# Score matmuls of a gated linear attention on 64x32 tiles of TensorE, keys in two parts, without the masked key part of the highest level

## What is computed

```python
def _attn_ref(q, k, v, alpha):
    for t in range(S):
        state = alpha[:, :, t, :, None] * state + np.einsum('bhd,bhe->bhde', k[:, :, t], v[:, :, t])
        y[:, :, t] = np.einsum('bhd,bhde->bhe', q[:, :, t], state)

def _moe_ref(x, domain_probs, w1, w2):      # 4 experts, 384 -> 1024 -> 384
    p = domain_probs / (domain_probs.sum(-1, keepdims=True) + 1e-09)
    for e in range(E):
        out += p[:, e:e + 1] * (np.maximum(x @ w1[e], 0.0) @ w2[e])

def _moe2_ref(x, w_in, w_out):              # 384 -> 2048 -> 384
    h = x @ w_in
    return (h * np.clip(h + 3.0, 0.0, 6.0) / 6.0) @ w_out
```

## Time and profile before

| what | value |
|---|---|
| time, three runs | 1381.57 us median (1380.89 to 1384.29) |
| the profiled execution's own time | 1382.56 us |
| its span in the profile | 1380.6 us |
| TensorE busy | 1356.1 us (98%), 13596 matmuls and as many weight loads |
| VectorE, ScalarE, GpSimd busy | 699.7, 534.8, 790.9 us (51%, 39%, 57%) |
| mean granted TensorE clock | 0.989 |
| DMA | 150.33 MB, mean 109 GB/s |

### The profile page before, as it was taken

The page is one execution under the profiler, slowest core; times in us unless marked ns, Lnnn a source line. Parts: engine busy times, 40 slices in busy tenths (PEclk is TensorE's granted clock), DMA queues, the critical chain, the costliest instruction groups (busy, mean ns, idle before and its releaser), DMA issues.

```text
span 1380.6 us, 34120 instructions
## 1 busy us (share of the span) xinstructions
PE 1356.1 (98%) x13596; PEld 1105.3 (80%) x13596; DVE 699.7 (51%) x1401; ACT 534.8 (39%) x992; POOL 790.9 (57%) x863
## 2 busy tenths in 40 slices
PE   6799999999999999999999999999999999999998
PEld 5578888888888888888888888888888888888887
DVE  8877665444454554454544544454445443333333
ACT  2233334333354333354433344533335433335543
POOL 7877665656565656565656565656564444444442
PEclk7899999999999999999999999999999999999999
DMA  4243343343334433433443334343322343333331
GB/s 146 73 144 119 115 117 117 104 125 95 110 96 126 126 118 103 119 95 114 130 126 104 109 96 126 104 124 112 114 85 85 99 128 106 104 99 92 99 118 35
DMA packets 70667, 150.33 MB, mean 109 GB/s; under 512 B 9584, under 2 KB 22128, under 8 KB 70512
## 3 DMA queue, kind: packets, MB, share of 16 engines
q1 hardware_dynamic: 70512, 148.16, 35.8%
HBM read 143.36 MB, written 4.77 MB: 107 GB/s over the span
## 4 chain that ended last, share of the span: by engine, by line
PE 95%; issue 0%; DVE 0%; ACT 0%; DVEq 0%
PE psum L517 43%; PE psum L501 42%; PE psum L417 5%; PE psum L458 1%; PE psum L438 1%; PE psum L428 1%; PE psum L473 1%; PE psum L481 1%; DVE result L664 0%; DVE psum L644 0%; DVE x_lo L660 0%; ACT gate L779 0%; ACT x_hi L799 0%; DVEq L148 0%; ACT w_hi L792 0%
## 5 line engine op out<-in xcount | busy, mean ns | idle before, releaser
L892 POOL TENSOR_TENSOR w_lo<-w_raw,w_hi 128x768 fp32r<-128x768 f32 (+1 forms) x291 | 531.7, 1828 | 537.2 <-ACT w_hi L792 537.2
L786 ACT ACTIVATE h_hi<-psum 128x512 fp32r<-128x512 f32 x288 | 172.6, 599 | 628.1 <-DVE psum L638 553.3
L517 PE MATMUL psum<-h_hi,w_hi 128*128 128x512 f32 x864 | 344.8, 399 | 0.2 <-DVE x_lo L660 0.2
L517 PE MATMUL psum<-h_hi,w_lo 128*128 128x512 f32 x864 | 337.3, 390 | 0.0
L501 PE MATMUL psum<-x_hi,w_hi 128*128 128x512 f32 x864 | 336.5, 389 | 0.3 <-issue 0.3
L517 PE MATMUL psum<-h_lo,w_hi 128*128 128x512 f32 x864 | 336.7, 390 | 0.0
L501 PE MATMUL psum<-x_lo,w_hi 128*128 128x512 f32 x864 | 336.1, 389 | 0.0
L501 PE MATMUL psum<-x_hi,w_lo 128*128 128x512 f32 x864 | 336.1, 389 | 0.0
L638 DVE SCALAR_TENSOR_TENSOR psum<-psum,probs 128x512 f32<-128x512 f32 x192 | 134.2, 699 | 349.4 <-PE psum L501 349.3
L792 ACT ACTIVATE w_hi<-w_raw 128x768 fp32r<-128x768 f32 x288 | 241.4, 838 | 0.0
L650 DVE TENSOR_TENSOR h_lo<-psum,h_hi 128x512 fp32r<-128x512 f32 x288 | 197.3, 685 | 46.5 <-ACT h_hi L786 46.5
(11 more groups left out here) (52 smaller groups left out, 717.4 us busy)
## 6 DMA issues: line engine op xcount, KB each, us to landing
w_raw<-w SPq DMA_DIRECT2D x288, 384.0 KB, 3.1
alpha_q<-qa SPq DMA_DIRECT2D x48, 256.0 KB, 3.8
k_raw<-kk SPq DMA_DIRECT2D x48, 128.0 KB, 3.7
probs<-prob_scratch SPq DMA_DIRECT2D x24, 256.0 KB, 3.6
v_diag<-v SPq DMA_DIRECT2D x96, 48.0 KB, 2.5
out<-result SPq DMA_DIRECT2D x18, 256.0 KB, 4.0
level_sb<-level SPq DMA_DIRECT2D x1, 80.0 KB, 3.2
ident_sb<-ident SPq DMA_DIRECT2D x1, 64.0 KB, 2.9
```

The costliest lines, as they stand in the source:

```text
L517: mm = pe.matmul(out_bank[k], a, x[:, g % DEEP, :], start=first and i == 0, stop=last and i == 2)
L786: act.activation(h_hi[:, g % DEEP, :], h_bank[g % 2][:, :], ACT.Copy).then_inc(hh_made, 1)
L892: op = pool.tensor_tensor(w_lo[:, g % RING, cols], w_raw[:, g % RAW, cols], w_hi[:, g % RING, cols].bitcast(F32), ALU.subtract)
```

## The change

In `score`, each matmul whose stationary operand was 64 keys becomes two, of 32 keys each, on the output quarters `quarter(jj, 0)` and `quarter(jj, 1)`: 64 rows by 32 columns of the array instead of 64 by 64, with the same moving operand. At level 5 the second part (keys 32 to 63, which the mask leaves out) is not made, from chunk 2 on; for chunks 0 and 1, the first to write the two pairs of banks, it is. A chunk has 88 score matmuls instead of 48 (96 in chunks 0 and 1). What `keep` reads is unchanged. Nothing else is edited.

```diff
                 for l in range(LEVELS):
                     at, width = ((0, CH // 2), (CH // 2, CH))[l] if l < 2 else (CH // 2 * (l + 1), CH // 2)
+                    parts = 2 if l < LEVELS - 1 or n < 2 else 1
                     for jp in range(2):
                         for i in range(2):
                             for jj in range(2):
...
                                 lo = 512 * i + SLAB * jp + at
-                                mm = pe.matmul(j_out[own(jj), lo:lo + width], k_level(n, l)[own(i), j, :], moving,
-                                               start=True, stop=True)
+                                for half in range(parts):
+                                    mm = pe.matmul(j_out[quarter(jj, half), lo:lo + width],
+                                                   k_level(n, l)[own(i), j, 32 * half:32 * half + 32], moving,
+                                                   start=True, stop=True)
                 mm.then_inc(p_made, 1)
```

## The result

The changed kernel takes **1455.7 us** (median of four runs, 1451.48 to 1460.06) against 1382.05 us in as many runs of the kernel before: a ratio of 1.053 (95% interval 1.051 to 1.055). It is slower, by 73.6 us. The profiled execution has a span of 1457.7 us, 77.1 more than before. The four runs fall in two pairs (1451.5 and 1451.9, 1459.6 and 1460.1 us), and the profiled one is of the upper pair, so sums from its trace come out some 4 us above the median.

The account below looks back on a forecast made before the run. The prediction took TensorE, busy 98% of the span, to bound the kernel. Against the profiled 1382.56 us it summed -8 + 39 + 20 + 6 = +57 to 1439.6, so 1438 us for the median, range 1400 to 1475.

Parts of the forecast that it names:

- pace of 40 bursts: Main loop score bursts: 176 records at 6.5 to 6.7 ns save 0.2 us per chunk, 40 chunks, -8 us.
- stops for code, main loop: Main loop: TensorE waits for code when two block borders lie in one score burst, +39 us (ends 27 and 51).
- half clock, main loop: Main loop: after each of 12 stops of 2 us or more, 3.4 us at half rate, +20 us (ends 0 and 41).
- prologue: Prologue: rounds grow from some 366 to 526 instructions; 1 us for each of six rounds, +6 us (ends 0 and 14).
- One block ahead and no more: TensorE's code fetch: the next 256-instruction block's packet starts only once the block before it is entered.
- the ramp: Main loop chunks 9, 13, 16, 28, 29, 41, 42: first border at position 101 to 131, partial stops of 0.8 to 2.3 us.
- code is fetched in time: Rival: no waits for code, only the pace is left, 1381.6 - 8 = 1373.6 us; chance 0.08.
- X: Time from entering a code block to using the next: taken as 4.2 us in the main loop, ends 3.5 and 5.0.
- VectorE and GpSimd and the filler matmuls hide much of it: Prologue: other work covers most of 8.4 us of code fetching a round, leaving 1 us for each of six rounds.
- 6.5 ns: Time per record read from L458's 32 records of 64x32 tiles in the main loop, applied to the new score bursts.
- the tile's columns set the pace: Score bursts: 64x32 tiles start records faster (6.5 ns) than 64x64 tiles (14.6 ns); moving columns do not matter.
- The tiles don't overlap in this order: Rival: four matmuls in a row on the same 64 rows, 13.3 ns a record, 2.3 us a burst, 1460 us; chance 0.08.

Follow-up runs that it names:

- e2: Changed kernel with 52 tiny matmuls on zeros (208 instructions) between prologue and main loop, moving only the code-block borders: 1425.2 us (one run).
- e3: Changed kernel with 20 tiny matmuls on zeros (80 instructions) between prologue and main loop, moving only the code-block borders: 1477.0 us (one run).
- e4: Changed kernel with 64x32 tiles only from chunk 8 on, the prologue's eight chunks as before the change: 1405.4 us (one run).
- e8: Changed kernel with the masked key part of the highest level computed as well, 192 records a burst: 1495.1 us (one run).
- e6: Changed kernel with the score burst cut in two around 18 large matmuls from chunk 16 on, earlier chunks on 64x64 tiles: 1400.2 us, ratio 1.0125.
- e5: Changed kernel with 64x32 tiles in the prologue's eight chunks alone, main loop on 64x64 tiles as before: 1401.6 us (one run).
- e7: Kernel before, with only the highest level on 64x32 tiles and its masked key part left out, from chunk 2 on: 1383.42 us, ratio 1.0006.
- e1: Changed kernel with the order inside a level turned so consecutive score matmuls alternate between the two row halves: 1461.66 us (one run).

## Why the prediction was right, and which terms were not

The direction and the cause held: 1438 us was said (the sum gives 1438.6) with 1400 to 1475, and 1455.7 came. The slowdown was put at 57 us and is 74. The two large terms, both of the main loop, were right; the other two missed by 14 and 15 us, both to the same side. Term by term, as the sum had them:

| term | said | measured | from |
|---|---|---|---|
| pace of 40 bursts | -8 | +6 | 1.68 us instead of 1.53, x 40 |
| stops for code, main loop | +39 | +36 | 16 gaps |
| half clock, main loop | +20 | +19 | 37.5 us at half rate |
| prologue | +6 | +21 | 94.5 instead of 73.7 us |

The measured ones add to 82, for 77 of the span; part of the low clock falls into stops, where it costs nothing. The same sum, with each run's own numbers, gives the main loop's extra time in the others (us over the 1301.9 of before):

| kernel | stops, over 1 us | stops, us | low clock, us | stops + half of it + burst | measured |
|---|---|---|---|---|---|
| changed | 13 | 35.8 | 37.5 | 60 | 56 |
| e2, moved by 208 | 4 | 10.3 | 10.2 | 21 | 20 |
| e3, moved by 80 | 20 | 50.4 | 41.0 | 77 | 73 |
| e4, main loop only | 4 | 9.3 | 13.7 | 22 | 22 |
| e8, masked part kept | 20 | 55.8 | 68.3 | 101 | 94 |

**Code: right.** One block ahead and no more, a stop when two borders lie in one burst, and the chunks by counting: 11, 15, 25 to 27 and 37 to 40 all have theirs, and of the seven on the ramp 13, 16, 28, 29, 41 and 42 do, the later ones in the turn or the large matmuls behind the burst. Chunk 9 has none and 14 has one of 0.9 us that was not named. The border is 256 instructions and not the work: e2, e3 and e4 moved the stops by count, and e6 removed them. One block ahead shows at all 16 stops: no further packet had started when TensorE went on, and the next one started 1.2 to 4.2 us later. By the rule set beside the rival "code is fetched in time" no burst of 352 would wait; in the main loop eight were cut. X, the time from entering a block to the use of the next, was near the middle: a full stop took 2.0 to 3.6 us where 3.2 was said. Its packet time of 1.65 us came from one packet; at these stops it was 0.9 to 1.4.

**Clock: right in sum.** Some stops over 2 us were followed by 3.4 us at 1.2 GHz, some by 6.8, and some, above all those near 2 us, by none. The term was half the stretch of one row of the prologue, and that it met is partly luck; e3 shows the spread.

**Prologue: the step that failed most.** It said that "VectorE and GpSimd and the filler matmuls hide much of it", 1 us a round. The stops fell in the scores, once a round, 2.1 to 4.4 us each, and e5 shows the price of the prologue alone, 19.3 us. The price of a stop stood in the same text, 3.2 us; seven of them are 22. The step should have asked what can run past a score that stands still: the filler matmuls are queued behind it on the same engine.

But the stops alone are not the bill. Before the change TensorE waited 8.0 us in the prologue's attends (L458 6.8, L473 1.2; 3.9 of it at borders), and 0.3 of that is left. Stretches of the prologue, before and after (columns as in the earlier trace rows):

```profile
0.00:73.73 73.73, 54.60 (x1460) 40.60 (x1461) 60.88 (x161) 18.31 (x59) 60.64 (x121) 0.79 0.37 108
0.00:94.47 94.47, 64.92 (x2133) 47.25 (x2133) 60.47 (x161) 18.55 (x59) 59.60 (x122) 0.66 0.28 86
```

TensorE's idle time rose by 10.4 us (19.1 to 29.5) and its busy time by 10.3. The same 68 filler matmuls are busy for 32.4 us instead of 25.8, and the mean granted clock is 0.66 instead of 0.79. The sum had a loss for the clock in the main loop alone. How much of the 10.3 is the clock stays open: in e5 the mean was 0.76, and the prologue ended only 1.5 us earlier.

**Pace: wrong in sign.** The step took L458's "6.5 ns" as a pace. Those 32 records are just as many as go fast at the start of any burst of such tiles here; the changed burst shows 5.5 ns over its first 32, some 11 over the next 35 and 8.5 over the last 109. From first start to last that is 1.55 us for 176 records, against 1.38 for 96 at 14.6 ns. The row was of the right tile and too short a burst. Narrower tiles did start faster, as "the tile's columns set the pace" had it, but not by enough for nearly twice as many records. So the change has nothing to win here even where the code is in time, as e6 and e7 show: by this sum the rival "code is fetched in time" would have ended at 1388 (1381.6 + 6), not at 1373.6.

**The nearest rival.** "The tiles don't overlap in this order" stood at 1460, nearer to 1455.7 than the forecast, and a burst longer than forecast was named as its sign. It is still out: it wanted bursts of 2.3 us, 1.68 came, and e1 changed nothing by alternating the row halves. The time alone would not have told the two apart.

## What to carry to other kernels

Cutting a matmul into smaller tiles multiplies instructions, and instructions have prices of their own: here a pace of 8.3 ns a record that narrower tiles did not beat, and blocks of code that must have been fetched. Count the instructions of the longest quick burst before counting array time; if it is longer than a block (here 352 against 256), the time depends on where the borders fall, and an edit anywhere ahead moves them. A price for a burst is read from one at least as long, and from its later part, not its start.

## What the runs showed of the hardware that was not expected

- Past the first 32, small matmul records started every 8.3 ns (4.2 ns an instruction) with 2 or 32 moving columns (e2, e3, the changed kernel), in either order of the row halves (e1). Before that, 5.5 to 6.5 ns.
- Where the borders of 256-instruction blocks fall was worth 52 us: 1425.2 us with 52 idle matmuls ahead of the main loop, 1477.0 with 20 (one run each).
- A block was in use 1.2 to 1.6 us after its packet had landed, at all stops of the changed kernel.
- Stops of 2.0 to 3.6 us were followed by a granted clock of 0.50 (1.2 GHz) for 3.4 us, for 6.8 us, or not at all. In the changed kernel all four of over 3 us were; in e1 one of 3.6 us was not.
